# Retention, channel MLP and spatial gating on one core: four changes of order around the second slot and the last turned half

## The reference

```python
# q, k, v: (2, 8, 768, 64)
for t in range(S):                       # S = 768
    state = gamma * state + k_t v_t^T    # per batch and head, gamma by head
    y[t] = q_t @ state / sqrt(64)
x  = y, heads side by side               # (2, 768, 512)
h  = (x^T @ U @ V)^T                     # U (768, 32), V (32, 768)
u  = x + h
x2 = u + relu(u @ w_ch1) @ w_ch2         # (512, 2048), (2048, 512)
a  = relu(x2 @ w_in)                     # (512, 1024)
uu, vv = a[:, :512], a[:, 512:]
out = (uu * (w_spatial @ normalise(vv) + b_spatial)) @ w_out
```

## Time and profile before

| | us |
|---|---|
| median of 3 runs | 485.77 (485.32 to 486.08) |
| the profiled execution | 485.74 |
| its span in the trace | 484.0 |
| PE busy | 475.5 (98%) |
| DVE, ACT, POOL busy | 202.4, 169.6, 101.9 |

### The profile page before, as it was taken

How to read it: one execution, slowest core, us unless ns; L and a number is a source line. 1 busy time by engine, 2 the same in 40 slices (tenths; PEclk the granted TensorE clock), 3 DMA queues, 4 the chain that set the end, 5 groups by cost and what they waited for, 6 DMA issues and landing times.

```text
span 484.0 us, 7201 instructions
## 1 busy us (share of the span) xinstructions
PE 475.5 (98%) x2744; PEld 405.7 (84%) x2744; DVE 202.4 (42%) x340; ACT 169.6 (35%) x301; POOL 101.9 (21%) x87
## 2 busy tenths in 40 slices
PE   8899989999999999999999999999999999999997
PEld 5688878888888888888888888888888889999997
DVE  4888886322326543222322541222321775521530
ACT  2534465323336424323333422323331652221212
POOL 2544531232222211232222111232222040000000
PEclk9999999999999999999999999999999999999999
DMA  8999952500000000000000005000002000011003
GB/s 283 373 292 322 323 221 98 250 0 0 0 1 1 0 1 0 0 0 0 0 1 2 0 1 216 12 0 0 0 0 88 0 1 1 1 65 66 0 1 130
DMA packets 8150, 33.30 MB, mean 69 GB/s; under 512 B 832, under 2 KB 2496, under 8 KB 5824
## 3 DMA queue, kind: packets, MB, share of 16 engines
q1 hardware_dynamic: 7712, 32.46, 18.2%
q10 hardware_dynamic: 416, 0.53, 0.3%
HBM read 29.84 MB, written 3.15 MB: 68 GB/s over the span
## 4 chain that ended last, share of the span: by engine, by line
PE 92%; DMA 4%; DVE 1%; SPq 1%; issue 0%; ACT 0%; DVEq 0%
PE bank L1042 10%; PE bank L954 9%; PE bank L955 9%; PE bank L956 9%; PE bank L943 9%; PE bank L944 9%; PE bank L945 9%; PE bank L1057 7%; DMA w2raw<-w 3%; PE bank L968 2%; PE bank L973 2%; PE bank L969 2%; PE bank L1000 2%; PE bank L999 2%; PE bank L998 2%; PE bank L826 2%
## 5 line engine op out<-in xcount | busy, mean ns | idle before, releaser
L340 POOL TENSOR_TENSOR w2l<-w2raw,w2h 128x512 fp32r<-128x512 f32 x48 | 63.7, 1327 | 214.7 <-ACT w2h L445 214.7
L682 DVE SCALAR_TENSOR_TENSOR hl<-bank,hh 128x512 fp32r<-128x512 f32 x48 | 33.2, 691 | 168.1 <-ACT hh L451 168.1
L943 PE MATMUL bank<-uth,w1h 128*128 128x512 f32 x192 | 74.9, 390 | 1.3 <-DVE utl L672 1.3
L945 PE MATMUL bank<-uth,w1l 128*128 128x512 f32 x192 | 74.7, 389 | 0.0
L944 PE MATMUL bank<-utl,w1h 128*128 128x512 f32 x192 | 74.7, 389 | 0.0
L954 PE MATMUL bank<-hh,w2h 128*128 128x512 f32 x192 | 74.7, 389 | 0.0
L955 PE MATMUL bank<-hl,w2h 128*128 128x512 f32 x192 | 74.7, 389 | 0.0
L956 PE MATMUL bank<-hh,w2l 128*128 128x512 f32 x192 | 74.7, 389 | 0.0
L451 ACT ACTIVATE hh<-bank 128x512 fp32r<-128x512 f32 x48 | 28.7, 598 | 89.0 <-PE bank L945 89.0
L445 ACT ACTIVATE w2h<-w2raw 128x512 fp32r (+1 forms) x48 | 30.2, 630 | 67.6 <-PE bank L956 66.3
L943 PEld LDWEIGHTS bank<-uth,w1h 128*128 128x128 f32 x192 | 36.0, 188 | 8.9 <-issue 1.5
(11 more groups left out here) (89 smaller groups left out, 679.8 us busy)
## 6 DMA issues: line engine op xcount, KB each, us to landing
att<-attn SPq DMA_DIRECT2D x7, 1152.0 KB, 7.8
w1raw<-w SPq DMA_DIRECT2D x4, 1024.0 KB, 7.8
w2raw<-w SPq DMA_DIRECT2D x4, 1024.0 KB, 9.2
att<-attn SPq DMA_DIRECT2D x10, 384.0 KB, 5.1
out_T<-stage SPq DMA_DIRECT2D x7, 384.0 KB, 2.3
winraw<-w_in SPq DMA_DIRECT2D x1, 2048.0 KB, 11.4
wsp_raw<-w_sp SPq DMA_DIRECT2D x1, 1920.0 KB, 7.4
tab<-decay SPq DMA_DIRECT2D x7, 258.0 KB, 4.1
```

What stands on the lines that cost most here:

```text
L340: nc.gpsimd.tensor_tensor(w2l[k][:, :], w2raw[:, f, :], raw(w2h[k])[:, :], ALU.subtract).then_inc(w2_lo, 1)
L682: nc.vector.scalar_tensor_tensor(out=hl[k][:, :], in0=hid_ps[k][:, :], scalar=0.0, in1=raw(hh[k])[:, :], op0=ALU.max, op1=ALU.subtract).th ...
L943: mm(hid_ps[k][:, :], w1h[k][:, s], uth[t % 2][:, c, :], start=(c == 0), stop=False)
L945: m = mm(hid_ps[k][:, :], w1l[k][:, s], uth[t % 2][:, c, :], start=False, stop=(c == CT - 1))
```

## The change

- SP issues the load of the identity ahead of slot 1's table, not behind it.
- ACT rounds U ahead of the copy of the second half of slot 1's scores, not behind it; DVE makes U's rest ahead of masking that half, not behind it.
- V's rest moves from DVE to POOL, where it stands behind `decays(2)` and waits for V's load, its rounding and the end of `decays(2)`. POOL's loop over the slots is written out, with constants in its waits.
- ACT rounds the first tile of the second weights behind both `xn_copy` of slot 7 and the last column block of u, not ahead of them.

```diff
             sp.wait_ge(qk_loaded[0], 16)
+            sp.dma_start(ident[:, :], eye).then_inc(eye_loaded, 16)
             load_tab(0, 1)
-            sp.dma_start(ident[:, :], eye).then_inc(eye_loaded, 16)
             sp.dma_start(urep[:, :, :], u_rep).then_inc(cst_loaded, 16)
...
             decays(1, 1, 0)
-            with pool.Fori(0, NI // 2 - 1) as j:
-                mask_b(2 * j + 1, 1)
-                decays(2 * j + 2, 0, j + 1)
-                mask_b(2 * j + 2, 0)
-                decays(2 * j + 3, 1, j + 1)
+            for i in range(1, NI - 1):
+                mask_b(i, i % 2)
+                decays(i + 1, (i + 1) % 2, (i + 1) // 2)
+                if i == 1:
+                    pool.wait_ge(vraw_loaded, 16)
+                    pool.wait_ge(v_hi, 1)
+                    pool.wait_ge(k_decayed, i + 2)
+                    nc.gpsimd.tensor_tensor(vst[R:2 * R, :], vraw[R:2 * R, :], raw(vst)[R:2 * R, :],
+                                            ALU.subtract).then_inc(v_lo, 1)
+                    pool.wait_ge(v_lo, 1)
...
                 xn_copy(i - 1, 1)
-                sc_copy(i, 1)
                 if i == 1:
                     act.wait_ge(cst_loaded, 16)
                     nc.scalar.activation(ust[:, :, :], urep[:, :, :], ACT.Copy).then_inc(ust_hi, 1)
+                sc_copy(i, 1)
                 p_round(i - 1)
...
             xt_copy(NI - 1, 1, 1)
-            round_w2(0, 0, 0)
             xn_copy(NI - 1, 0)
             split_u(0, range(3, 4))
             xn_copy(NI - 1, 1)
+            round_w2(0, 0, 0)
...
                 xn_rest(i - 1, 1)
-                mask_a(i, 1, k, pair)
                 if i == 1:
                     dve.wait_ge(cst_loaded, 16)
                     dve.wait_ge(ust_hi, 1)
                     nc.vector.tensor_tensor(ust[:, :, 3 * R:P], urep[:, :, 3 * R:P], raw(ust)[:, :, 3 * R:P],
                                             ALU.subtract).then_inc(ust_lo, 1)
+                mask_a(i, 1, k, pair)
                 states(i, 0, NC - 2, k)
                 states(i, NC - 2, NC - 1, k)
                 p_rest(i - 1)
-                if i == 1:
-                    dve.wait_ge(vraw_loaded, 16)
-                    dve.wait_ge(v_hi, 1)
-                    nc.vector.tensor_tensor(vst[R:2 * R, :], vraw[R:2 * R, :], raw(vst)[R:2 * R, :],
-                                            ALU.subtract).then_inc(v_lo, 1)
                 decay_q(i + 1, 1 - k, (i + 1) // 2)
```

## The result

The changed kernel takes 487.95 us in the median of 20 runs (484.86 to 488.97), the kernel before 486.07 in 20 runs beside it. The ratio is 1.0035, with an interval of 1.002 to 1.0049: slower by a third of a percent. That lies inside the stated range, 485.1 to 488.0, by 0.05 us and by luck: the range was drawn without the falling clock, and ten of the 20 runs lie above it. The likeliest case was 486.5. The rival of the falling clock came true, to which the prediction gave 12%.

The account below looks back on a forecast made before the run. PE, busy 98% of the span, was taken as the bound. 485.74 + 1.95 (V's rest) - 1.03 (second weights) = 486.66, or 486.02 with POOL undisturbed; forecast 486.5, own range 485.9 to 487.0, stated range 485.1 to 488.0.

Parts of the forecast that it names:

- stated range: Whole kernel: 485.1 to 488.0 us, leaving out the fallen clock and the early transfer.
- likeliest case: Whole kernel: forecast of 486.5 us, own range 485.9 to 487.0, given 66%.
- The rival of the falling clock: PE in slot 2: long gap before `up(0)` lowers PE's clock, about 2.1 us lost, 488.7 us; chance 12%.
- V's rest on POOL: Slot 2: `up(0)` waits for POOL until 24.83 or 24.19; second scores 1.95 us later, or 1.31 with POOL undisturbed.
- The second weights: Last quarter of the first hidden tile: ACT's wait for their load no longer delays block 3 of u, 1.03 us gained.
- U ahead: Slot 1: PE's wait for U's rest goes, outputs end about 0.7 us earlier; no gain unless `up(0)` can start.
- The identity: Slot 1: its issue ahead delays the table by 0 to 0.43 us, taken as 0.2, without effect on the end.
- The early transfer: Rival, slot 2: table lands 1.6 us sooner, at 18.9, because slot 3's q and k are issued later; 484.4 us; chance 8%.
- the cheap subtraction: Rival, V's rest in slot 2: POOL's subtraction takes 0.95 us instead of 1.83, giving 485.7 us; chance 6%.
- the empty edit at the end: Rival, second weights' move: brings nothing because another releaser of block 3 stands right behind, 487.5 us; chance 5%.
- the three waits that it names: PE before 72 us: 1.3 us at first hidden tile's last quarter, 1.2 at first product with U, 1.0 at second scores.

Follow-up runs that it names:

- the fastest version: Changed kernel with V's rest on POOL ahead of the decays of slot 2 and the identity's load behind slot 1's table again: 482.76 us, ratio 0.993.
- the filled kernel: Changed kernel with three idle products of 512 columns on PE ahead of `up(0)` in slot 1: 485.95 us, ratio 1.0008.
- the profile of 0.996: Profiled execution of the changed kernel in its first set, unedited, named by its mean granted clock: 488.63 us.
- a kernel with a gap of 2.4 us: Changed kernel with two idle products of 512 columns on PE ahead of `up(0)`: 487.05 us, ratio 1.0015.

## Why the prediction was right or wrong, step by step

**V's rest on POOL: right in place and cause, near in size.** It predicted `up(0)` at 24.83 or 24.19 and a gap of 3.5 to 4 us; `up(0)` came at 24.40 after 3.64. In its profile POOL's decays went first (1.53 us), DVE's queries beside them took 2.20 and ended at 22.60, and POOL's subtraction took 2.17 from 22.09, where it takes 1.80 alone (the fastest version), for the predicted 1.83. Decays, queries and subtraction one after another, as the prediction has it, would end at 22.60 + 1.80 = 24.40; the subtraction ended at 24.26. So adding up was right to 0.14 us. Of the 0.43 us by which `up(0)` came before 24.83, 0.27 are POOL's earlier start (20.39 for 20.66, since the table landed earlier), and the rest is this overlap. With the clock up, in the filled kernel, the second scores start at 26.55, 1.45 us later than before, for the predicted 1.31 to 1.95, and 2.19 us behind `up(0)`, for 2.22.

**The second weights: right.** 0.97 us in the profile and 1.1 alone, for 1.03. What the prediction did not see is that this wait is also a place where the clock can fall.

**U ahead: right for this change, and it had a value of its own.** The prediction gave the 0.7 us as worth nothing unless `up(0)` can start, and behind a V rest that waits for the table it is worth nothing. With V's rest on DVE the profiles show 0.6 to 0.7 us gained at the second scores of slot 2. Whether the gains of the two good edits add is open. Measured alone they are 1.1 and 1.1 us, and both together, with the identity ahead and V's rest on DVE, 1.2; but that last figure is 0.8 to 2.1 by its interval. Its profile, taken of a run of 484.10, shows 0.67 at slot 2 and 71.88 - 70.24 = 1.64 us at the last quarter of the first hidden tile, so there they do add.

**The identity: not measured.** The whole times can't tell 0 to 0.43. The profiles hint at a price: from the first to the second scores of slot 1 it is 1.72 to 2.23 us in the five with the identity behind the table (the kernel before among them), and 2.12 to 3.67 in the seven with it ahead, where two stand above 3.6. These are single executions, so it stays open.

**The falling clock: the step that failed is its chance.** The mechanism was written down with its size (5 us of work at the ratio 1.75, 2.1 us), but at 12% and with a point of decision near 4 us. It fell in 30 of 32 runs, in a kernel whose two profiles have gaps of 3.6 and 3.9 us, and in 10 of 12 at 2.9. The stated range, too, was drawn as if it would not fall. The size was a guess in the right region: the 5 us stood on no row, and the windows show 0.36 + 2 + 1.08 = 3.4 us at half clock in the profile of 0.996, and 1.04 + 4 + 1.8 = 6.8 us in that of 0.993. At the ratio of 1.75 these would cost 1.5 and 2.9 us (an estimate). Filling the gap took the ratio from 1.0035 to 1.0008. Without this price the likeliest case would have stood: 1.0008 x 486.07 = 486.5, and the two groups of runs lie 1.1 and 2.4 us above that. What in the profile of before could have warned is the start: there the lower level shows in durations, 1.65 us for the scores, though the granted clock reads 1.00 (window 4 to 6). Nothing there tells how long a gap is enough, and so a gap three times the longest one seen should not have been given one chance in eight. The page of the Trainium skill that the prediction cited, "TensorE: Matmul & The Clock Gate", section "What's actually happening", says that the slow state is the default and activity releases it. The traces agree: 1.65 us for the first scores of the kernel before and 0.94 for those of its later slots, and 1.65 again behind the idle gap of the changed kernel.

**The early transfer, the cheap subtraction, the empty edit at the end** did not happen: the table landed 6.68 us after its issue for 7.08, at 20.32; the subtraction cost its length; the last edit paid in full. One reading was off, without effect: beside the three waits that it names, PE's list of waits outside the start has one lesser one (0.7 us), not two.

## What to carry to other kernels

A wait on PE costs its length and can cost the clock behind it, the more often the longer it is: here a kernel with a gap of 2.4 us ahead of dense work lost it in 7 of 12 runs. Before an operation is moved to an idle engine, look at what stands ahead of it in that engine's queue: POOL was idle for 2.3 us right where V's rest was needed, and the same instruction one place earlier turned a loss of 0.35% into a gain of 0.7% (six runs). Where a gap can't be closed, products without use can fill it: here three of them did, and one or two left the clock falling in half of the runs. And when an edit lets PE arrive earlier at a wait that something else ends, the gap there grows.

## What the runs showed of the hardware that was not expected

The clock falls after gaps well under 3 us, but not each time: 7 of 12 runs at 2.4 us, and profiles with 1.93 and 1.90, but not one with 1.87. It can fall late: in the changed kernel's profile about 1.2 us after PE had resumed (0.91 over 24 to 26), in its second one already during the gap (0.74 over 22 to 24). The kernel before has such runs as well, 19 of 81, with a median 1.0 us higher (486.66 for 485.68); those with U ahead and V's rest in time have 3 of 36, the one with only the second weights moved 1 of 12. A POOL subtraction on 32 partitions costs the time of its 768 elements a partition: 1.80 us, where the line through the operations on 128 partitions gives 1.83.
